# Where TensorE's operands begin, and how free expert slots are filled: attention, MLP and routed MLP in one kernel

## The reference

```
scores  = scale * x @ state.T ; a  = softmax(scores)  ; xread = a @ state      # 8 batches, 8 heads, 512 tokens, 32 states, D = 64
scores2 = scale * state @ x.T ; a2 = softmax(scores2) ; sread = a2 @ x
x = concat([xread, sread], axis=2)            # 8 * (512 + 32) = 4352 rows of 512
h = x @ w_in ; x = max(0.01 * h, h) @ w_out   # 512 -> 2048 -> 512
logits = x @ w_gate ; e_idx = argmax(logits)  # 8 experts
out[e] = gate_w * sigmoid(x @ w_output_gate)[e] * (relu(x[e] @ w1[e]) @ w2[e])   # 512 -> 1024 -> 512
```

## The kernel before, in words

| matmuls | tiles | before | after |
|---|---|---|---|
| up, 768 x 512 columns | v, aT | 0, 0 | 0, 32 |
| down, 1632 x 512 | gT, wout | 32, 0 | 0, 32 |
| experts' first product, 1536 x 256 | w1, xgT | 0, 32 | 0, 32 |
| experts' second product, 888 x 512 | hT, w2 | 32, 0 | 0, 32 |
| first product of a step of one tile, 120 x 512 | xgT, w1 | 32, 0 | 32, 0 |
| state rows' up, 192 x 256 | wch, sr | 32, 32 | 0, 0 |
| v of each batch, 512 small ones | stT, win | 32, 0 | 32, 32 |

## Time and profile before

### The profile page before, as it was taken

One profiled execution on the slowest core, in us unless ns is written; L12 is line 12 of the kernel. 1 busy time (PEld: TensorE's weight loads), 2 busy tenths in 40 slices (PEclk: granted clock), 3 DMA queues, 4 the chain that ended last, 5 costly groups with the idle time before them and its releaser, 6 DMA issues.

```text
span 1160.9 us, 18319 instructions
## 1 busy us (share of the span) xinstructions
PE 1122.3 (97%) x6514; PEld 899.8 (78%) x6515; DVE 625.3 (54%) x1378; ACT 400.8 (35%) x752; POOL 215.7 (19%) x307
## 2 busy tenths in 40 slices
PE   5999999999999999999999999799999999989995
PEld 2777777777776777777777889688998989878884
DVE  6584573764854845737645577373332336366332
ACT  4344334434433443344343444141221124244211
POOL 1000011020020110200200323532231233333321
PEclk9999999999999999999999999899999999999998
DMA  9611120120120111200132111971111124543110
GB/s 343 247 53 37 37 78 1 41 73 1 42 73 4 66 46 37 79 1 1 37 73 73 55 38 43 318 206 40 54 54 36 45 64 87 158 108 115 39 55 19
DMA packets 39250, 86.41 MB, mean 74 GB/s; under 512 B 11173, under 2 KB 12453, under 8 KB 39080
## 3 DMA queue, kind: packets, MB, share of 16 engines
q1 hardware_dynamic: 24712, 47.70, 13.8%
q0 software_dynamic: 14480, 37.94, 10.3%
HBM read 63.47 MB, written 28.87 MB: 80 GB/s over the span
## 4 chain that ended last, share of the span: by engine, by line
PE 86%; DVE 5%; DMA 4%; issue 2%; POOL 1%; ACT 1%; DVEq 0%; POOLq 0%; SPq 0%; ACTq 0%
PE bank L508 27%; PE bank L510 26%; PE bank L509 26%; PE bank L541 2%; DMA y_buf<-w_out_dram 2%; PE bank L575 1%; PE bank L559 1%; DMA rows_dram<-w_hi,odd_i 1%; PE bank L583 1%; PE bank L519 1%; PE bank L548 1%; POOL rows_dram L414 0%; DVE v_lo L1163 0%; DMA s_in<-rows_dram 0%; PE bank L792 0%
## 5 line engine op out<-in xcount | busy, mean ns | idle before, releaser
L508 PE MATMUL bank<-wout_lo,gT_hi 128*128 128x512 f32 x544 | 218.0, 401 | 0.0
L509 PE MATMUL bank<-wout_hi,gT_lo 128*128 128x512 f32 x544 | 214.9, 395 | 0.0
L510 PE MATMUL bank<-wout_hi,gT_hi 128*128 128x512 f32 x544 | 214.3, 394 | 0.0
L1181 DVE TENSOR_TENSOR g_buf<-g_buf,bank 128x512 f32<-128x512 f32 (+1 forms) x144 | 94.2, 654 | 108.8 <-ACT g_buf L934 108.7
L508 PE MATMUL bank<-xgT_lo,w_hi 128*128 128x256 f32 x512 | 146.6, 286 | 5.4 <-DVE xgT_lo L1330 2.8
L509 PE MATMUL bank<-xgT_hi,w_lo 128*128 128x256 f32 x512 | 145.8, 285 | 0.0
L510 PE MATMUL bank<-xgT_hi,w_hi 128*128 128x256 f32 x512 | 145.8, 285 | 0.0
L396 POOL DMA_INDIRECT rows_dram<-y_buf,row_i x34 | 35.1, 1032 | 545.8 <-DVE row_i L1274 538.2
L934 ACT ACTIVATE g_buf<-bank 128x512 f32<-128x512 f32 (+1 forms) x144 | 82.5, 573 | 152.4 <-PE bank L510 151.3
L1185 DVE TENSOR_TENSOR gT_lo<-g_buf,gT_hi 128x512 fp32r<-128x512 f32 (+1 forms) x144 | 95.4, 663 | 72.9 <-ACT gT_hi L940 71.4
L940 ACT CAST gT_hi<-g_buf 128x512 fp32r<-128x512 f32 (+1 forms) x144 | 85.9, 597 | 134.9 <-DVE g_buf L1181 130.5
(11 more groups left out here) (233 smaller groups left out, 1760.0 us busy)
## 6 DMA issues: line engine op xcount, KB each, us to landing
xq<-rows_dram POOLq DMA_DIRECT2D x88, 128.0 KB, 3.0
raw<-w_dram SPq DMA_DIRECT2D x20, 512.0 KB, 8.4
raw<-w_dram SPq DMA_DIRECT2D x10, 1024.0 KB, 10.6
X<-x_in_dram SPq DMA_DIRECT2D x8, 1024.0 KB, 7.2
XT<-xT_in_dram SPq DMA_DIRECT2D x7, 1024.0 KB, 5.6
rows_dram<-x_in_dram SPq DMA_DIRECT2D x1, 4128.0 KB
win<-w_in_dram SPq DMA_DIRECT2D x4, 1024.0 KB, 12.3
y_buf<-w_out_dram POOLq DMA_DIRECT2D x6, 512.0 KB, 8.4
```

What stands on the lines that cost most here:

```text
L508: pe.matmul(o, l_hi, r_lo, start=first, stop=False)
L509: pe.matmul(o, l_lo, r_hi, start=False, stop=False)
L510: return pe.matmul(o, l_hi, r_hi, start=False, stop=last)
L1181: dve.tensor_tensor(g_buf[:, n, 0:w], g_buf[:, n, 0:w], up_b[n][:, 0:w], ALU.max).then_inc(g_ready, 1)
```

## The change

1. *Layout.* Tiles are placed so that the classes of the last column above come out: the arena is rounded up to 64 bytes, aT, win and wout (now one tile) are shifted by 32, and so are w2 and xgT. To make room const loses columns that repeated themselves (262 to 214 floats; VectorE now reads w8 and e34 by a broadcast), the integer tiles of the routing become one, and the buffer of loaded rows is 4096 bytes long instead of 4128.
2. *Constants.* They come in three transfers, behind the first piece of win, behind the second, and behind X. TensorE and VectorE wait for all three.
3. *Fill.* `fill_tails` issues two scatters. The first has one run of 16 rows (33,024 bytes) on each of 128 partitions, 16 runs per expert; runs that would begin at or behind the expert's next multiple of 256 rows get a place beyond the end and are dropped. The second writes single rows up to the next multiple of 16. The source is wout. The wait is for 32 instead of 144.
4. *Order on VectorE.* `fill_rows`, now 23 instructions on one or eight columns instead of 13, stands behind `rows_lo(1)` instead of ahead of `plan_order`.

```diff
-        arena = cursor[0]
+        arena = -(-cursor[0] // 64) * 64
+        def home(place):
+            cursor[0] = arena + place
+        home(0)
         v_hi = [at(f"v_hi{n}", [P, 2, VW], f32r) for n in range(2)]
         v_lo = [at(f"v_lo{n}", [P, 2, VW], f32r) for n in range(2)]
+        home(16384 + 32)
         aT_hi = [at(f"aT_hi{n}", [P, 2, S], f32r) for n in range(2)]
...
-        wout_hi = at("wout_hi", [P, F1, DM], f32r)
-        wout_lo = at("wout_lo", [P, F1, DM], f32r)
+        wout = at("wout", [P, 2, F1, DM], f32r)
+        wout_hi, wout_lo = wout[:, 0], wout[:, 1]
...
         for s in range(2):
+            home((65536 + 64) * s)
             w1_hi.append(at(f"w1_hi{s}", [P, DC, FF2], f32r))
             w1_lo.append(at(f"w1_lo{s}", [P, DC, FF2], f32r))
+            cursor[0] += 32
             w2_hi.append(at(f"w2_hi{s}", [P, F2, DM], f32r))
...
+        filler = wout[:, :, :, :].bitcast(fp32).rearrange("p i f n -> p (i f n)")[:, 0:GROUP * ROW]
...
-        layer_at = cursor[0]
+        cursor[0] = layer_at = -(-(cursor[0] + 32) // 64) * 64
...
-        cursor[0] = layer_at
+        cursor[0] = layer_at - 32
         xgT_hi = at("xgT_hi", [P, DC, PAIR], f32r)
         xgT_lo = at("xgT_lo", [P, DC, PAIR], f32r)
+        cursor[0] += 32
         hT_hi = at("hT_hi", [P, F2, PAIR], f32r)
...
-            sp.dma_start(const[:, :], consts).then_inc(const_in, 16)
             load_win(0)
+            sp.dma_start(const[:, K_ID:K_W8 + E], consts[:, C_ID:C_W8 + E]).then_inc(const_in, 16)
             load_win(1)
+            sp.dma_start(const[:, K_TOK:K_END], consts[:, C_TOK:C_END]).then_inc(const_in, 16)
             load_x(0)
+            sp.dma_start(const[:, K_E34:K_E34 + E], consts[:, C_E34:C_E34 + E]).then_inc(const_in, 16)
             load_stT(1)
...
-                some_rows = w1_hi[0][:, :, :].bitcast(fp32).rearrange("p k f -> p (k f)")
-                for e in range(E):
-                    pool.indirect_dma_start(out=rows_dram.rearrange("(a two) n -> a (two n)", two=2),
-                                            out_offset=bass.IndirectOffsetOnAxis(ap=fill_i[:, e:e + 1], axis=0),
-                                            in_=some_rows[:, 0:2 * ROW], in_offset=None,
-                                            bounds_check=SLOTS // 2 - 1, oob_is_err=False).then_inc(filled, 16)
-                pool.indirect_dma_start(out=rows_dram, out_offset=bass.IndirectOffsetOnAxis(ap=odd_i[:, 0:1], axis=0),
-                                        in_=some_rows[:, 0:ROW], in_offset=None,
+                pool.indirect_dma_start(out=rows_dram.rearrange("(a g) n -> a (g n)", g=GROUP),
+                                        out_offset=bass.IndirectOffsetOnAxis(ap=fill_i[:, 0:1], axis=0),
+                                        in_=filler[:, :], in_offset=None,
+                                        bounds_check=SLOTS // GROUP - 1, oob_is_err=False).then_inc(filled, 16)
+                pool.indirect_dma_start(out=rows_dram, out_offset=bass.IndirectOffsetOnAxis(ap=fill_i[:, 1:2], axis=0),
+                                        in_=filler[:, 0:ROW], in_offset=None,
                                         bounds_check=SLOTS - 1, oob_is_err=False).then_inc(filled, 16)
...
-            pe.wait_ge(const_in, 16)
+            pe.wait_ge(const_in, 48)
...
-            fill_rows()
             plan_order()
             plan_steps()
...
             rows_lo(1)
+            fill_rows()
             dve.wait_ge(o_ready, 2)
```

More of the change, by code:

```diff
@@ L127, in build @@
         top, gate, z, ez, ebase, rankf, colf, posf, tokf = (r_small[:, 4 * n:4 * n + 4] for n in range(9))
[L128 to L131, removed]
+        r_int = at("r_int", [P, 16], i32)
+        rank_i, col_i, pos_i, tok_i = (r_int[:, 4 * n:4 * n + 4] for n in range(4))
         assert cursor[0] <= nc.sbuf_usable_end, cursor[0] - nc.sbuf_usable_end
@@ L1288, in route_slots @@
                 if state:
[L1289 removed]
+                    dve.tensor_copy(tok_i[:, 0:T], const[:, K_TOKS:K_TOKS + 2])
                 else:
@@ L1296, in route_slots @@
                 step.end()
-            w8_row = const[0:1, C_W8:C_W8 + E]
+            w8_row = const[0:1, K_W8:K_W8 + E]
             def choose_first():
@@ L1470, in fill_rows @@
             def fill_rows():
-                count, away = before[:, 2, :], float(2 * SLOTS)
-                step(dve.tensor_scalar(end_half_i[:, :], count, 1.0, None, ALU.add))
-                step(dve.tensor_scalar(end_half_i[:, :], end_half_i[:, :], 1, None, ALU.logical_shift_right))
-                step(dve.tensor_copy(end_half[:, :], end_half_i[:, :]))
-                dve.scalar_tensor_tensor(odd_at[:, :], end_half[:, :], 2.0, count, ALU.mult, ALU.subtract)
-                step(dve.tensor_scalar(fill_at[:, :], end_half[:, :], const[:, C_TOK:C_TOK + 1], None, ALU.add))
@@ L1483, in fill_rows @@
-                step(dve.tensor_tensor(odd_at[:, :], odd_at[:, :], ident[:, 0:E], ALU.mult))
-                step(dve.reduce_sum(odd_f[:, :], odd_at[:, :], AX.X))
-                dve.tensor_scalar(odd_i[:, :], odd_f[:, :], away, None, ALU.add).then_inc(fill_ready, 1)
+                assert E * GROUP == P and PAIR == GROUP * GROUP
+                away = float(2 * SLOTS)
+                count, group, end, at_group, at_row, far_group, far_row = (fill_f[:, n:n + 1] for n in range(7))
+                grp, mine, group0, row0, nth = (fill_f[:, n:n + 1] for n in range(7, 12))
@@ new lines, in fill_rows @@
+                step(dve.tensor_copy(fill_n[:, 4:5], const[:, K_TOK:K_TOK + 1]))
+                step(dve.tensor_scalar(fill_n[:, 5:6], fill_n[:, 4:5], 4, None, ALU.logical_shift_right))
+                step(dve.tensor_copy(nth, fill_n[:, 5:6]))
+                dve.scalar_tensor_tensor(grp, nth, -float(GROUP), const[:, K_TOK:K_TOK + 1], ALU.mult, ALU.add)
+                dve.tensor_scalar(group0, nth, float(CPE * P // GROUP), None, ALU.mult)
+                dve.tensor_scalar(row0, nth, float(CPE * P), None, ALU.mult)
@@ new lines, in fill_rows @@
+                step(dve.tensor_scalar(mine, nth, float(CPE), None, ALU.mult))
+                step(dve.tensor_scalar(fill_sel[:, :], const[:, K_E34:K_E34 + E], mine, None, ALU.is_equal))
+                step(dve.tensor_tensor(fill_sel[:, :], before[:, 2, :], fill_sel[:, :], ALU.mult))
+                step(dve.reduce_sum(count, fill_sel[:, :], AX.X))
+                dve.tensor_scalar(fill_n[:, 0:1], count, float(GROUP - 1), None, ALU.add)
+                step(dve.tensor_scalar(fill_n[:, 1:2], count, float(PAIR - 1), None, ALU.add))
@@ new lines, in fill_rows @@
+                dve.tensor_scalar(fill_n[:, 2:3], fill_n[:, 0:1], 4, None, ALU.logical_shift_right)
+                step(dve.tensor_scalar(fill_n[:, 3:4], fill_n[:, 1:2], 8, None, ALU.logical_shift_right))
+                step(dve.tensor_copy(fill_f[:, 1:3], fill_n[:, 2:4]))
+                dve.tensor_tensor(at_group, group, grp, ALU.add)
+                step(dve.tensor_tensor(at_row, count, grp, ALU.add))
+                dve.scalar_tensor_tensor(far_group, end, float(PAIR // GROUP), at_group, ALU.mult, ALU.is_le)
@@ L1487, in plan_order @@
+                dve.scalar_tensor_tensor(far_row, group, float(GROUP), at_row, ALU.mult, ALU.is_le)
+                dve.tensor_tensor(at_group, at_group, group0, ALU.add)
+                step(dve.tensor_tensor(at_row, at_row, row0, ALU.add))
+                dve.scalar_tensor_tensor(fill_i[:, 0:1], far_group, away, at_group, ALU.mult, ALU.add)
+                dve.scalar_tensor_tensor(fill_i[:, 1:2], far_row, away, at_row, ALU.mult, ALU.add).then_inc(fill_ready, 1)
             def plan_order():
@@ L1501, in plan_order @@
                 dve.tensor_tensor(place[0][:, 8:16], some[:, :], rest[:, :], ALU.mult)
-                step(dve.tensor_tensor(base_of[:, :], some[:, :], const[0:1, C_E34:C_E34 + E], ALU.mult))
+                step(dve.tensor_tensor(base_of[:, :], some[:, :], const[0:1, K_E34:K_E34 + E], ALU.mult))
                 step(dve.tensor_copy(counts[:, :], counts_i[:, :]))
```

41 lines of the change are left out of this document (19 added, 22 removed).

## The result

The changed kernel took 1172.49 us (median of four runs, 1172.34 to 1172.67) against 1163.95 for the kernel before beside it: a ratio of 1.0073, 95% interval 1.0056 to 1.0091. It is 8.5 us slower; forecast were 22.7 us faster, and the range, which began at 1125, ended at 1167.

The account below looks back on a forecast made before the run. TensorE's matmul spacing and stops were taken to bound the kernel. Layout -24.0, constants +1.0 and scatters +0.3 gave -22.7 us, from a median of 1163.66 to 1141.0; range 1125 to 1167.

Parts of the forecast that it names:

- Layout, -24.0 us forecast: Down, second product and up: closer matmul spacing from the new tile places saves 20.9 plus 3.1 us.
- 225.0 ns: Spacing forecast for 512-column matmuls in down, up and second product: 213.3 + 11.7, between bounds 213.3 and 236.8.
- The first product's 11.7 ns: Experts' first product, 256 columns: loss per matmul beyond its columns, assumed to belong to the weight load at any width.
- 24 ns more for a group beside which the next weights are loaded: Packed matmul groups of 512 and 256 columns: read as a weight-load cost of 24 ns, the same for either width.
- Rival 2: Matmul spacings stay as they were and only 1.3 us of costs remain: 1165 us; chance 0.13.
- Constants, +1.0 forecast: Start of the first layer: TensorE waits for the third constants transfer behind X, costing about 1.0 us, bounds 0.3 to 3.0.
- fill_rows moved, TensorE 5.1 us further: Second expert step: starts 2.1 us sooner and probably spares 3.05 us of half clock, a lead lost in the later wait.
- covered: VectorE behind fill_rows: o_buf's second half and s_now, needed at 742 at the earliest, would be ready in time.
- The scatters, +0.3 forecast: Second expert step: TensorE's restart after the third step's rows comes 0.3 us later, at 757.0; range -5 to +2.9.
- shared equally: Fill against SP's weights: sharing 320 GB/s evenly, the fill's 2.05 MB need 12.8 us and land at 747.7.
- The forecast landing, 746.6: Last fill scatter: lands at 746.6, taken near the even split, with 741.3 if alone and 749.1 behind all weights.
- rival 5: The fill piles up on few transfer engines, landing at 752; restart moves by 5.7 us: 1147 us; chance 0.07.

Follow-up runs that it names:

- b_all0: The kernel before with layer_at rounded up to 64 bytes, so all four products have weights and streamed tiles at 0; 1155.78 us, ratio 0.9927.
- fill_spread: The changed kernel with only the partitions of the fill's groups changed, at most five groups per transfer engine; 1169.31 us, ratio 1.0045.
- fill_early: The changed kernel with fill_rows moved back ahead of plan_order, the two scatters of 16-row groups staying; 1169.76 us, ratio 1.0045.
- fill_both: The changed kernel with fill_rows ahead of plan_order and the fill's groups spread over the partitions; 1160.18 us, ratio 0.9966.

## Why the prediction was wrong

*Layout, -24.0 us forecast, +2.1 in the layers and +0.7 in the expert steps measured.* The step that failed is "all have weights at 0 and streamed tiles at 32, the classes that only the first product has today", and with it 225.0 ns. It took the places modulo 64 for the cause, because the change was told in them. What counts is the distance between the two tiles over 256 bytes. Down went from -32 to -96 and the second product from -32 to -96 or +96, all between 233.2 and 234.2 ns; up, the one product at distance 0, was moved off it and lost 3.7 ns x 768 = 2.8 us. Rows that could have warned stood in the prediction: the earlier trace rows had the closest spacing of all, and up was the only product of 512 columns whose tiles were equal; the prediction explained this by the weights' class, one of two readings that its rows allowed. The first product's 11.7 ns were carried to 512 columns as a cost per weight load. At distance 0 that is right (the commonest spacing, 226.7 ns, and 120.0 are 544 and 288 cycles at 2.4 GHz, 32 more than the columns at either width); at -96 it is not: 120.0 ns are 32 cycles more than the columns, 233.3 ns are 48. Nor do show what was read in them, 24 ns more for a group beside which the next weights are loaded. The view from which their second line comes goes on:

```profile
L583 PEld LDWEIGHTS bank<-scT,wg x8: 110/110/110, 518.5 to 518.7; 128*32 128x32 f32 x8
L583 PE MATMUL bank<-scT,wg x8: 379/379/379, 518.7 to 518.9; 128*32 128x256 f32 x8
```

These weights were loaded while the yT matmuls of 518.5 and the first scT matmuls of 518.7 ran, and both groups took 379 ns; only the first group, at 518.2, took 403. So the reason for taking 225.0 out of 213.3 to 236.8 was a misreading.

*Rival 2, no effect on spacing*, came true in size but not by its reason. The Trainium skill, "TensorE: Matmul & The Clock Gate", Part 2, says in its first step that loading weights doesn't steal read bandwidth from the running matmul. These runs speak against it: b_all0 moves tiles by 32 bytes, leaves the instructions as they are, and shortens the spacing of 1632 matmuls by 5 ns each, so it matters where the weights' tile and the streamed tile begin to each other. That the two reads meet is still an inference; the runs show the dependence and not the mechanism.

*Constants, +1.0 forecast, 1.3 measured.* Right in place and kind. const landed at 21.1, not 20.2, because X's own issue moved from 4.12 to 4.96, with two transfers of constants ahead of it instead of one, which the prediction had counted as hidden.

*fill_rows moved, TensorE 5.1 us further.* The second step did start without a wait, 3.0 us sooner than before (733.27 against 732.88 + 3.4, by which the layers were late), and 735 to 741 ran at full clock. But "covered" was wrong for what stands behind it on VectorE. fill_rows ended at 736.4 instead of the 733.8 + 3.4 = 737.2 of the forecast, the o_buf half behind it at 737.1; then came 3.43 us that the profile calls issue. By the code what stands there is the entry into the loop of expert steps; ScalarE's first hidden part had been ready since 735.3. Before, these lay in a pause of 7.71 us. Now the first hidden rest of the second step was made at 740.80, TensorE stood idle for 2.22 us before it could go on, and half the clock went with it, 3.4 us at 0.50: 3.9 us of the lead were gone. They cost nothing in the end, since TensorE came to the third step's rows too early all the same and waited 13.60 us.

*The scatters, +0.3 forecast, 6.1 measured.* The start was forecast well (734.1 + 3.4, measured 737.34). What failed is "shared equally", in two ways. The runs did not move beside the first four weight transfers: their first packet began at 744.35, 7.0 us behind the issue, as the last packet of those four ended (744.38). Beside the last two, which landed at 752.0 and 761.8, they did move. And the sum took all engines as equally loaded, while from 744.35 on eight runs in a row on one engine took 10.9 us. fill_spread puts a size to the second: 3.4 us of landing. The forecast landing, 746.6 + 3.4 of lateness = 750.0, was missed by 6.3 us, so some 2.9 us are left for the first. Why the runs waited is open; the scatters of the kernel before, in packets of 4 KB, moved beside the same four transfers (both ended at 744.9). The pile-up is rival 5, with +5.7 at a chance of 0.07. The prediction had the formula and had counted the 62 uneven groups, and the row against it ("all 128 runs of a scatter were equal before") was no evidence, since equal runs cannot show it.

*The numbers.* Two rivals came true at once, each on a part that the other does not touch: 1165 with the 0.3 of the fill replaced by rival 5's 6.0 is 1170.7, within 1.8 us of the result. That it comes so close is partly luck: rival 5 had the weights share the engines from 734.9 on and had no part for the 7.0 us in which the runs did not move. The range treated rivals as alternatives to each other and so ended at the larger of them. Independent parts want their cases added.

Left open: by what mechanism the distance acts, why its sign matters (229.4 at -64, 233.5 at +64), +32 at 512 columns and -32, +64 and 128 at 256, which no run had, and whether a longer period than 256 would show at more than the one distance tried.

## What to carry to other kernels

Before a tile's alignment is named as a cause, list every pair of tiles (weights and streamed) with its measured spacing, and test the difference of the two addresses as well as each one's value; one run that shifts everything alike and one that shifts one side tell them apart. For indirect scatters, spread the live runs over the partitions so that each transfer engine gets its share, and when work is moved on an engine, look for the next thing that is needed behind it, loop entries included. When a change has independent parts, let the range hold the sum of their bad cases.

## What the runs showed of the hardware

Float32r matmuls of 512 columns, each with its own weights, are spaced 226.9 to 234.2 ns in the mean, depending on where the two tiles stand to each other over 256 bytes; for 256 columns 117.3 to 120.0, and the good distances differ: 0 is best for the one and among the worst for the other. The single spacings follow a pattern that repeats within a block and from layer to layer (231, 232, 237 in the changed kernel's down; 234, 231, 235, 233 before). One run of 33,024 bytes took 1.22 us in the median of the changed kernel's trace, 27 GB/s on its engine, and 2.43 at most in fill_early. Row loads that landed after 4.2 us took 11.5 in fill_early and 10.6 in fill_both, where most of SP's 4.2 MB of weights was still to move when they were issued.
